# Both tiles' probabilities turned in one go, and small operations moved from VectorE to GpSimd, in an attention and MLP kernel

## The chip, the cores and the metric

One core of one Trainium2 chip runs the whole program. The metric is the device time of an execution in microseconds (us). Engines are PE (TensorE), VectorE (DVE in the rows), ScalarE (ACT), GpSimd (POOL) and SyncE (SP), which starts most transfers.

## The reference

```
scores = q @ k^T / 8                      # 4 batches x 8 heads, 576 x 576, head size 64
mask   = scores >= 32nd largest of the row
attn   = softmax(where(mask, scores, -1e9))
x      = (attn @ v) as 2304 tokens x 512
x      = softplus(x @ w_in) @ w_out       # 512 -> 2048 -> 512
logits = x @ w_gate                       # 8 experts, the largest one is taken
out    = gate * (relu(x @ w1[e]) @ w2[e]) # 512 -> 1024 -> 512 for the tokens of e
```

All of it is float32. Products whose result must be exact enough are made of three matmuls of a high and a low part of each operand (hi x hi, hi x lo, lo x hi); the low part is what is left when the rounded high part is subtracted.

## The kernel before, in words

Attention is cut into 72 blocks. A full block holds 128 queries of a pair of heads, so it has two tiles t = 0, 1 of 128 x 576 scores; a block of the kind "ends" collects the last 64 rows of two batches. Each engine has its program written out by hand, in steps i. In step i PE makes the scores of block i + 1, turns the probabilities of block i - 2 (transposes through PSUM, `turn_probs`) and multiplies them with v (`times_v`). VectorE finds the 32 largest values of block i by four rounds of MAX8 with a MATCH_REPLACE8 in between (`maxima`, `strike`) and makes the reciprocals of the softmax denominators (`reciprocals`). GpSimd masks block i - 1: one tile takes two operations (L1479, L1482), the other takes one on ScalarE (L848) and one on GpSimd (L1475). ScalarE copies scores out of PSUM (`scores_out`), takes exponentials (`exponentials`, L855), normalises (L861) and copies the turned tiles (`probs_out`, L868) and the product with v (`x_out`, L875), which is the high part of x; VectorE subtracts it from the PSUM value for the low part (`x_low`, L1128).

From step 10 (MLP_AT) to step 73 the first MLP runs beside attention: a group of 256 tokens takes eight units, one a step. `up` makes 256 features (24 matmuls, L598 to L600), ScalarE takes the absolute value, the rectified value and a logarithm (L883 to L892), GpSimd adds them (`softplus`, L1487), ScalarE copies the high part (`h_high`, L900), GpSimd subtracts for the low part (`h_low`, L1493), and in the next step `down` multiplies with w_out in two halves of six matmuls (L617 to L619). When a group is through, ScalarE empties the two banks of down (`down_out`), and in two steps of the next group (TURNS) PE turns a tile of tokens (`turn_tokens`) and computes its logits (`logits`), both in bank 5, which `up` uses too; `up` of the next step waits until the logits have been copied.

PSUM has 8 banks of 512 columns. Scores of a tile lie as two halves of 288 columns in two banks, four banks in all; the turned probabilities of one tile (640 columns) lie in the upper part of banks 0 to 4, the product with v in bank 4. There is room for one turned tile, so PE turns t = 0, makes half of down, waits for ScalarE's copy, and turns t = 1. After step 73 come the last MLP group, routing and the experts.

What orders the work is the sequence of calls in each engine's program; between engines stand semaphores.

Of the kernel before, what the change touches and what calls it, by code (L numbers as in the profile page):

```python
# [20 lines left out]
def build(nc, q, k, v, w_in, w_out, w_gate, w1, w2, out):  # L21
# [62 lines left out]
    TURNS = {}  # L84
# [32 lines left out]
    with ExitStack() as ctx:  # L117
# [35 lines left out]
        prT = phase("prT", [P, FULL + 1, 2, P])  # L153
# [3 lines left out]
        top = phase("top", [P, 6, TOPK])  # L157
        bias = phase("bias", [P, 2, 2, 2])
        den = phase("den", [P, 2, 2])
        rden = phase("rden", [P, 2, 2])  # L160
        phase("gap_b", [P, WLEN - 4 * PAIRS * SEQ // 2 - PAIRS * (FULL + 1) * P - 6 * TOPK - 3 * 8])
# [116 lines left out]
        first_scores = sem("first_scores")  # L278
# [5 lines left out]
        transit_full, transit_copied = sem("transit_full"), sem("transit_copied")  # L284
        pv_ready, x_copied, x_split = sem("pv_ready"), sem("x_copied"), sem("x_split")
# [48 lines left out]
        def x_source(n):  # L334
            raw = psum[:, 4, 0:P]
            return raw if PLAN[n][0] == "full" else raw.rearrange("p (t q) -> p t q", t=2)
# [173 lines left out]
        def _(pe):  # L510
            turns = 0

            def scores(n):
# [6 lines left out]
                if n >= 4:  # L520
                    pe.wait_ge(transit_copied, 2 * (n - 3))

                order = [(0, 0), (1, 0), (0, 1), (1, 1)] if n == 0 else [(0, 0), (0, 1), (1, 0), (1, 1)]
                for part, t in order:
                    keys = slice(part * HALF, (part + 1) * HALF)
                    for h in range(2):
# [7 lines left out]
                        mm = nc.tensor.matmul(psum[rows, 2 * part + t, 0:HALF],  # L534
                                              qT[h * HD:(h + 1) * HD, p, cols],
                                              kT[h * HD:(h + 1) * HD, p, keys],
                                              start=True, stop=True)
                    if n == 0 and (part, t) == (1, 0):
                        mm.then_inc(first_scores, 1)
                mm.then_inc(scores_ready, 1)  # L540

            def turn_probs(n, t):
                pe.wait_ge(pr_ready, 2 * n + t + 1)
                if n or t:
                    pe.wait_ge(transit_copied, 2 * n + t)
                if t == 0:
                    pe.wait_ge(scores_copied, 2 * min(n + 4, BLOCKS))
                if n and t == 0:
                    pe.wait_ge(x_copied, n)
                    pe.wait_ge(x_split, n)  # L550
                for c, keys in enumerate(KEYS):
                    mm = nc.tensor.transpose(transit[0:keys, c, :],  # L552
                                             pr[:, n % 2 * 2 + t, c * P:c * P + keys], ident[:])
                mm.then_inc(transit_full, 1)

            def times_v(n):
# [4 lines left out]
                pe.wait_ge(transit_copied, 2 * n + 2)  # L561
                for t, p in enumerate(pairs_of(n)):
                    for c, keys in enumerate(KEYS):
                        for h in range(2):
                            if kind == "full":
                                cols, probs = slice(0, P), prT[0:keys, c, h, :]
                            else:
                                cols = slice(t * HD, (t + 1) * HD)
                                probs = prT[0:keys, c, t, h * HD:(h + 1) * HD]
                            mm = nc.tensor.matmul(psum[h * HD:(h + 1) * HD, 4, cols],  # L570
# [3 lines left out]

            def up(g, u, amid=()):
                n = UNITS * g + u

                steps_x = PAIRS * 2 * (g + 1)
                k_last = KD - 1 if PIECES[2 * g + 1][0] == "full" else KD // 2
# [6 lines left out]
                if turns:  # L586
                    pe.wait_ge(logits_copied, turns)
                ps = psum[:, 5, 0:2 * WIDE].rearrange("p (a c) -> p a c", a=2)
                for part in range(2):
                    f = slice(part * P, (part + 1) * P)  # L590
                    for kk in range(KD):
                        if (part, kk) in amid:
                            amid[part, kk]()
                        if u == 0 and (part, kk) == (0, k_last):
                            pe.wait_ge(x_split, steps_x)
# [27 lines left out]
            def turn_tokens(g, kk, bank):  # L623
                pe.wait_ge(y_copied, kk + 1)
# [1009 lines left out]
```

## Time and profile before

| what | value |
| --- | --- |
| median of 3 runs | 1081.61 us (1079.75 to 3335.12) |
| the profiled execution | 1081.47 us |
| its span, first to last instruction | 1079.7 us |
| mean granted PE clock | 0.975 of full speed |
| PE, weight loads | 1006.0 us (93%), 810.3 us (75%) |
| VectorE | 842.9 us (78%) |
| ScalarE | 738.1 us (68%) |
| GpSimd | 651.6 us (60%) |

The busy times are unions over the whole span. The span has an opening without the MLP (to about 113 us), the stage with attention and MLP together (to about 768 us), and the last MLP group with routing and experts. So a share of the whole says little about one stage.

### The profile page before, as it was taken

To read this page: it belongs to the slowest core of one execution; us is meant where nothing else is said; L and a number is where in the kernel's file an instruction comes from. 1 tells how busy PE (TensorE), PEld (TensorE's weight loads), DVE (VectorE), ACT (ScalarE), POOL (GpSimd) and SP (SyncE) were. 2 spreads that over 40 slices of the span, in tenths; PEclk is the share of its full clock that TensorE was granted. 3 is DMA by queue.
4 is the path that set the end of the run, shared out by engine and by line. 5 is a ranking of instruction groups with operands and counts; after the bars stand their busy time and mean duration, and the time that the engine had idled before them with its cause. 6 is when DMAs were issued, how large, how long until landed. Compare 5 with 4: busy or idle time off the path is not lost.

```text
span 1079.7 us, 21621 instructions
## 1 busy us (share of the span) xinstructions
PE 1006.0 (93%) x6951; PEld 810.3 (75%) x6952; DVE 842.9 (78%) x1879; ACT 738.1 (68%) x1391; POOL 651.6 (60%) x624
## 2 busy tenths in 40 slices
PE   3566899999999999999999999999999999999996
PEld 1344678887787787787778887787887788888875
DVE  7999999999999999999999999997154622222261
ACT  2887788988988988988888988988646121111140
POOL 2678687777777877878868778778443302211101
PEclk9966899999999999999999999999999999999999
DMA  9623126343234443332444323233482331111100
GB/s 321 239 87 140 70 96 205 121 140 118 98 118 154 161 126 125 116 118 86 152 150 152 119 102 118 98 119 117 139 325 102 121 125 41 49 48 39 39 19 19
DMA packets 42110, 130.46 MB, mean 121 GB/s; under 512 B 4064, under 2 KB 17376, under 8 KB 31776
## 3 DMA queue, kind: packets, MB, share of 16 engines
q1 hardware_dynamic: 38976, 119.57, 31.4%
q0 software_dynamic: 3040, 9.70, 2.6%
q8 instruction: 52, 0.85, 0.3%
q14 instruction: 42, 0.34, 0.1%
HBM read 111.43 MB, written 18.09 MB: 120 GB/s over the span
## 4 chain that ended last, share of the span: by engine, by line
PE 52%; POOL 25%; ACT 10%; issue 9%; DMA 1%; SPq 1%; DVE 1%; ACTq 0%; POOLq 0%; DVEq 0%
POOL pr L1479 7%; PE psum L690 6%; PE psum L692 6%; PE psum L691 6%; PE psum L570 6%; POOL pr L1482 5%; POOL h_lo L1493 4%; PE psum L534 4%; POOL hs L1487 4%; POOL pr L1475 4%; PE psum L552 4%; PE psum L598 3%; PE psum L617 3%; PE psum L619 3%; PE psum L618 2%
## 5 line engine op out<-in xcount | busy, mean ns | idle before, releaser
L1116 DVE MAX8 top<-work 128x8 f32<-128x576 f32 x432 | 305.1, 748 | 0.0
L1122 DVE MATCH_REPLACE8 work<-top,work 128x576 f32<-128x576 f32 x288 | 212.0, 744 | 0.0
L598 PE MATMUL psum<-x_parts,wi_hi 128*128 128x256 f32 x576 | 170.8, 296 | 0.0
L1487 POOL TENSOR_TENSOR hs<-hs,ab 128x512 f32<-128x512 f32 x72 | 92.9, 1290 | 124.1 <-ACT ab L892 124.1
L599 PE MATMUL psum<-x_parts,wi_hi 128*128 128x256 f32 x576 | 163.5, 284 | 0.0
L600 PE MATMUL psum<-x_parts,wi_lo 128*128 128x256 f32 x576 | 163.5, 284 | 0.0
L1479 POOL TENSOR_SCALAR pr<-sc,top 128x576 f32<-128x576 f32 x64 | 142.6, 2228 | 6.4
L552 PE MATMUL psum<-ident,pr 128*128 128x128 f32 (+1 forms) x720 | 109.3, 285 | 37.2 <-ACT prT L868 16.2
L552 PEld LDWEIGHTS psum<-ident,pr 128*128 128x128 f32 (+1 forms) x720 | 77.4, 139 | 69.5 <-issue 69.5
L598 PEld LDWEIGHTS psum<-x_parts,wi_hi 128*128 128x128 f32 x576 | 110.7, 192 | 25.2 <-issue 23.8
L855 ACT ACTIVATE pr<-pr,bias 128x576 f32<-128x576 f32 x144 | 111.1, 772 | 26.9 <-POOL pr L1482 25.9
L570 PE MATMUL psum<-prT,vtok 128*64 128x128 f32 (+3 forms) x1600 | 117.1, 287 | 10.2 <-ACT prT L868 10.1
L617 PE MATMUL psum<-wo_ring,h_hi 128*128 x288 | 124.2, 431 | 1.0 <-POOL h_lo L1493 0.8
L1475 POOL TENSOR_TENSOR pr<-sc,pr 128x576 f32<-128x576 f32 x80 | 113.8, 1426 | 17.1 <-ACT pr L848 17.1
L570 PEld LDWEIGHTS psum<-prT,vtok 128*64 128x64 f32 (+1 forms) x1600 | 85.7, 144 | 50.6 <-issue 31.9
L534 PE MATMUL psum<-kT,qT 64*128 64x288 f32 (+1 forms) x640 | 110.4, 468 | 9.8 <-ACT sc L840 9.0
L619 PE MATMUL psum<-wo_ring,h_lo 128*128 x288 | 113.8, 395 | 0.0
L1577 POOL DMA_INDIRECT out<-ys,dst_now x19 | 19.2, 1012 | 156.6 <-DVE ys L1323 155.6
L618 PE MATMUL psum<-wo_ring,h_hi 128*128 x288 | 113.2, 393 | 0.0
L599 PEld LDWEIGHTS psum<-x_parts,wi_hi 128*128 128x128 f32 x576 | 111.0, 193 | 0.2
L600 PEld LDWEIGHTS psum<-x_parts,wi_lo 128*128 128x128 f32 x576 | 110.9, 193 | 0.0
L868 ACT COPY prT<-psum 128x640 f32<-128x640 f32 x144 | 99.7, 693 | 12.8 <-PE psum L552 12.8
(205 smaller groups left out, 2192.4 us busy)
## 6 DMA issues: line engine op xcount, KB each, us to landing
wo_ring<-wo_parts SPq DMA_DIRECT2D x72, 1024.0 KB, 4.9
wo_parts<-wo_ring SPq DMA_DIRECT2D x8, 1024.0 KB, 3.9
kT<-in_k SPq DMA_DIRECT2D x16, 288.0 KB, 3.6
qT<-in_q SPq DMA_DIRECT2D x16, 288.0 KB, 4.6
vtok<-in_v SPq DMA_DIRECT2D x16, 256.0 KB, 2.8
wo_raw<-in_moe_w_out SPq DMA_DIRECT2D x1, 4096.0 KB, 14.8
wi_raw<-in_moe_w_in SPq DMA_DIRECT2D x4, 1024.0 KB, 13.7
x_rows<-x2tok SPq DMA_DIRECT2D x16, 256.0 KB, 2.4
```

Of the source, the lines that this page charges most:

```text
L534: mm = nc.tensor.matmul(psum[rows, 2 * part + t, 0:HALF], qT[h * HD:(h + 1) * HD, p, cols], kT[h * HD:(h + 1) * HD, p, keys], start=True, ...
L552: mm = nc.tensor.transpose(transit[0:keys, c, :], pr[:, n % 2 * 2 + t, c * P:c * P + keys], ident[:])
L570: mm = nc.tensor.matmul(psum[h * HD:(h + 1) * HD, 4, cols], vtok[0:keys, p, c, h * HD:(h + 1) * HD], probs, start=(c == 0), stop=(c == FULL))
L598: nc.tensor.matmul(ps[:, part, :], wi_hi[:, u, kk, f], hi, start=first, stop=False)
L599: nc.tensor.matmul(ps[:, part, :], wi_hi[:, u, kk, f], lo, start=False, stop=False)
L600: mm = nc.tensor.matmul(ps[:, part, :], wi_lo[:, u, kk, f], hi, start=False, stop=last)
L617: nc.tensor.matmul(psum[:, 6 + a, :], high, hi, start=(f == 0), stop=False)
L619: mm = nc.tensor.matmul(psum[:, 6 + a, :], low, hi, start=False, stop=(f == KF - 1))
L1116: nc.vector.max(top[:, at, 8 * r:8 * r + 8], sc[:, at, :] if r == 0 else work[:, t, :]).then_inc(topk_step, 1)
L1122: nc.vector.match_replace(work[:, t, :], top[:, at, 8 * r - 8:8 * r], sc[:, at, :] if r == 1 else work[:, t, :], TAKEN).then_inc(topk_step, 1)
L1475: nc.gpsimd.tensor_tensor(to, sc[:, at, :], to, ALU.subtract).then_inc(masked, 1)
L1479: nc.gpsimd.tensor_scalar(to, sc[:, at, :], top[:, at, TOPK - 1:TOPK], OUT, ALU.is_lt, ALU.mult).then_inc(mask_step, 1)
```

## The change

- PSUM: a tile's scores are now 512 columns in a bank of its own (banks 0 and 1), and the last 64 keys of both tiles lie together in the first 128 columns of bank 2 (`ends`). The turned probabilities of both tiles (1280 columns) lie without a gap in banks 2 to 4, and the product with v in the last 128 columns of bank 4.
- PE turns both tiles one behind the other and then makes both halves of down. ScalarE copies both turned tiles in one instruction.
- The tokens are turned in bank 0 and the logits made in bank 1, in steps of their own: two tiles take four steps. In the first step of a group the scores stand in the middle of `up`.
- ScalarE copies the product with v to a buffer in SBUF (`xraw`), at the start of the next step; GpSimd makes the high part by a copy and the low part by a subtraction (`x_split_up`).
- The sum of the two parts of a denominator goes to GpSimd from block 9 on (`denominators`); the reciprocal stays on VectorE, one round of MAX8 later.
- ScalarE takes both exponentials behind the logarithm.
- The first block's scores are no longer copied in a separate first half.

```diff
-        transit = psum[:, 0:FULL + 1, HALF:HALF + P]
+        ends = psum[:, 2, 0:2 * REST]
+        transit = psum[:, 2:5, :].rearrange("p b c -> p (b c)")[:, P:P + 2 * (FULL + 1) * P]
+        x_raw_at = psum[:, 4, 3 * P:4 * P]
+        chunks = transit.rearrange("p (t c q) -> p t c q", t=2, c=FULL + 1)
...
-            TURNS[up_step(g) + UNITS + 1 + a] = (g, 2 * g + a)
+            TURNS[up_step(g) + UNITS + 1 + 2 * a] = (g, 2 * g + a)
+            LOGITS[up_step(g) + UNITS + 2 + 2 * a] = 2 * g + a
...
                 if late:
-                    turn_probs(i - 2, 0)
+                    turn_probs(i - 2)
+                if i in TURNS:
+                    turn_tokens(*TURNS[i], 0)
+                if i in LOGITS:
+                    logits(LOGITS[i], 1)
                 if down_at(i):
-                    down(*down_at(i), 0)
-                if late:
-                    turn_probs(i - 2, 1)
-                if i in TURNS:
-                    turn_tokens(*TURNS[i], 5)
-                if down_at(i):
-                    down(*down_at(i), 1)
+                    for part in range(2):
+                        down(*down_at(i), part)
                 if late:
                     times_v(i - 2)
-                if i in TURNS:
-                    logits(TURNS[i][1], 5)
...
+            def x_split_up(n):
+                pool.wait_ge(x_copied, n + 1)
+                g = PLAN[n][4] // 2
+                if g >= 2:
+                    pool.wait_ge(h_raw, UNITS * (g - 1))
+                nc.gpsimd.tensor_copy(x_place(0, n), x_source(n)).then_inc(x_hi_ready, 1)
+                pool.wait_ge(x_hi_ready, n + 1)
+                nc.gpsimd.tensor_tensor(x_place(1, n), x_source(n), x_place(0, n).bitcast(F32),
+                                        ALU.subtract).then_inc(x_split, 1)
+
+            def denominators(n):
+                pool.wait_ge(exp_ready, 2 * n + 2)
+                if n >= 2:
+                    pool.wait_ge(rden_ready, n - 1)
+                nc.gpsimd.tensor_tensor(den[:, n % 2, :], eps[:, n % 2, :, 0], eps[:, n % 2, :, 1],
+                                        ALU.add).then_inc(den_step, 1)
...
+                if i >= MLP_AT and is_block(i - 3):
+                    x_split_up(i - 3)
                 if up_at(i - 1):
                     h_low(*up_at(i - 1))
...
+                if is_block(i - 1) and i - 1 >= MLP_AT - 1:
+                    denominators(i - 1)
```

## Rows read from the trace of the kernel before

**Rows 1.** Busy time of each engine by stage, with granted clock and transfers.
```profile
core 0: us, PE busy (x) PEld busy (x) DVE busy (x) ACT busy (x) POOL busy (x), PEclk, DMA share, GB/s
118.00:750.00 632.00, 620.85 (x4934) 502.15 (x4933) 619.32 (x1408) 559.47 (x1086) 494.68 (x430) 1.00 0.36 124
311.91:393.64 81.73, 80.22 (x619) 64.81 (x618) 80.89 (x185) 72.93 (x143) 64.47 (x57) 1.00 0.41 139
```

**Rows 2.** Timeline of VectorE: start and duration in us, line, operation.
```profile
370.38 1.41 DVE L1116 MAX8 top<-work 128x8 f32<-128x576 f32 x2
...
380.03 0.15 DVE L1133 TENSOR_REDUCE den<-eps 128x2 f32<-128x4 f32 x1
380.21 0.17 DVE L1136 RECIPROCAL rden<-den 128x2 f32<-128x2 f32 x1
380.29 0.27 DVE L1128 TENSOR_TENSOR x_parts<-psum,x_parts 128x128 fp32r<-128x128 f32 x1
380.48 1.41 DVE L1116 MAX8 top<-work 128x8 f32<-128x576 f32 x2
```

**Rows 3.** Timeline of PE's matmuls, one step with tokens and logits.
```profile
298.60 1.24 PE L534 MATMUL psum<-kT,qT 64*128 64x288 f32 x8
...
302.75 0.71 PE L552 MATMUL psum<-ident,pr 128*128 128x128 f32 x5
303.22 0.48 PE L617 MATMUL psum<-wo_ring,h_hi 128*128 x1
303.54 0.39 PE L618 MATMUL psum<-wo_ring,h_hi 128*128 x1
...
304.46 0.40 PE L619 MATMUL psum<-wo_ring,h_lo 128*128 x1
304.77 0.74 PE L552 MATMUL psum<-ident,pr 128*128 128x128 f32 x5
305.35 0.60 PE L628 MATMUL psum<-ident,x2tok 128*128 128x128 f32 x4
305.71 0.48 PE L617 MATMUL psum<-wo_ring,h_hi 128*128 x1
...
307.27 1.46 PE L570 MATMUL psum<-prT,vtok 128*64 128x128 f32 x20
308.66 1.06 PE L638 MATMUL psum<-wg,x2T 128*128 128x8 f32 x8
309.65 1.24 PE L534 MATMUL psum<-kT,qT 64*128 64x288 f32 x8
```

**Rows 4.** Timeline of GpSimd, one step; in brackets the idle time before and its releaser.
```profile
403.69 2.23 POOL L1479 TENSOR_SCALAR pr<-sc,top 128x576 f32<-128x576 f32 x1
406.00 1.43 POOL L1482 TENSOR_TENSOR pr<-pr,sc 128x576 f32<-128x576 f32 x1
407.38 1.44 POOL L1475 TENSOR_TENSOR pr<-sc,pr 128x576 f32<-128x576 f32 x1
410.24 1.28 POOL L1487 TENSOR_TENSOR hs<-hs,ab 128x512 f32<-128x512 f32 x1 [1.42 <-ACT ab L892]
411.60 0.23 POOL L1465 TENSOR_SCALAR bias<-top 128x2 f32<-128x2 f32 x1
...
412.25 1.30 POOL L1493 TENSOR_TENSOR h_lo<-hs,h_hi 128x512 fp32r<-128x512 f32 x1
413.65 2.23 POOL L1479 TENSOR_SCALAR pr<-sc,top 128x576 f32<-128x576 f32 x1
```

**Rows 5.** Timeline of ScalarE in the same step.
```profile
407.52 0.78 ACT L855 ACTIVATE pr<-pr,bias 128x576 f32<-128x576 f32 x1 [0.51 <-POOL pr L1482]
...
408.30 0.67 ACT L868 COPY prT<-psum 128x640 f32<-128x640 f32 x1
...
411.55 0.62 ACT L900 CAST h_hi<-hs 128x512 fp32r<-128x512 f32 x1 [0.48 <-POOL hs L1487]
```

**Rows 6.** Waits of GpSimd from 118 to 750 us: total, times, longest.
```profile
POOL hs L1487 <- ACT ab L892: 100.9, 62, 2.9
```

**Rows 7.** Groups by line and shape: count, busy us, mean ns, idle before.
```profile
L1509 POOL TENSOR_SCALAR_AFFINE_SELECT ident<-ident 128x128 f32<-128x128 f32 x1 | 0.3, 288 | 0.2 <-POOL ident L1507 0.2
L1504 POOL TENSOR_TENSOR wi_lo<-wi_raw,wi_hi 128x1024 fp32r<-128x1024 f32 x8 | 18.9, 2364 | 0.0
```

More of the change, by code:

```diff
@@ L510, in _ @@
         def _(pe):
-            turns = 0
+            turns, logit_turns = 0, 0
             def scores(n):
@@ L520, in scores @@
                 if n >= 4:
[L521 to L525, printed above, removed]
+                    pe.wait_ge(transit_copied, n - 3)
+                if turns:
+                    pe.wait_ge(turn_copied, turns)
+                if logit_turns:
+                    pe.wait_ge(logits_copied, logit_turns)
+                for last, t in ((True, 0), (False, 1), (False, 0), (True, 1)):
+                    keys = slice(FULL * P, SEQ) if last else slice(0, FULL * P)
+                    to = ends[:, t * REST:(t + 1) * REST] if last else psum[:, t, :]
+                    if last and t:
+                        pe.wait_ge(ends_begun, n + 1)
                     for h in range(2):
@@ L533, in scores, with turn_probs @@
                             rows = slice(h * HD, (h + 1) * HD)
[L534 to L535 removed]
+                        mm = nc.tensor.matmul(to[rows, :], qT[h * HD:(h + 1) * HD, p, cols],
                                               kT[h * HD:(h + 1) * HD, p, keys],
                                               start=True, stop=True)
[L538 to L539 removed]
+                    if last and t == 0:
+                        mm.then_inc(ends_begun, 1)
                 mm.then_inc(scores_ready, 1)
[L542 to L548, printed above, removed]
[L549 to L554 removed]
+            def turn_probs(n):
+                if n:
+                    pe.wait_ge(transit_copied, n)
+                    pe.wait_ge(x_copied, n)
+                pe.wait_ge(scores_copied, 2 * min(n + 4, BLOCKS))
+                for t in range(2):
+                    pe.wait_ge(pr_ready, 2 * n + t + 1)
+                    for c, keys in enumerate(KEYS):
+                        mm = nc.tensor.transpose(chunks[0:keys, t, c, :],
+                                                 pr[:, n % 2 * 2 + t, c * P:c * P + keys], ident[:])
+                    mm.then_inc(transit_full, 1)
             def times_v(n):
@@ L573, in times_v, with k_last @@
                 mm.then_inc(pv_ready, 1)
+            def k_last(g):
+                return KD - 1 if PIECES[2 * g + 1][0] == "full" else KD // 2
             def up(g, u, amid=()):
@@ L593, in up @@
                             amid[part, kk]()
-                        if u == 0 and (part, kk) == (0, k_last):
+                        if u == 0 and (part, kk) == (0, k_last(g)):
                             pe.wait_ge(x_split, steps_x)
@@ L1007, in _ @@
                         exponentials(i - 1, 0)
-                    if late:
-                        probs_out(i - 2, 1)
-                    if now:
                         exponentials(i - 1, 1)
@@ L1018, in _ @@
                     h_high(*up_at(i - 1))
+                if is_block(i - 3):
+                    x_out(i - 3)
+                if now:
+                    for t in cuts(i - 1):
+                        cut_off(i - 1, t)
                 if is_block(i + AHEAD):
-                    scores_out(i + AHEAD, 0)
-                    scores_out(i + AHEAD, 1)
+                    scores_out(i + AHEAD)
                 if late:
@@ L1024, in _ @@
                     normalise(i - 2, 1)
-                if now:
-                    for t in cuts(i - 1):
-                        cut_off(i - 1, t)
                 if up_at(i):
@@ L1030, in _ @@
                 if late:
-                    probs_out(i - 2, 0)
-                if now and i < BLOCKS:
-                    exponentials(i - 1, 0)
-                if late:
-                    probs_out(i - 2, 1)
-                if now and i >= BLOCKS:
-                    exponentials(i - 1, 0)
+                    probs_out(i - 2)
                 if i in TURNS:
-                    turn_out(TURNS[i][1], 5)
+                    turn_out(TURNS[i][1], 0)
+                if i in LOGITS:
+                    logits_out(LOGITS[i], 1)
                 if up_at(i):
```

117 lines of the change are left out of this document (56 added, 61 removed).

## The prediction

> **What bounds the kernel now.** I read the table by stage first, because the shares of the whole span mix three stages. In the stage in which attention and the first MLP run together (118 to 750 us) VectorE is busy 619.32 of 632 us, PE 620.85, ScalarE 559.47, GpSimd 494.68, with the clock at 1.00 (2.4 GHz) throughout [rows 1]. So two engines are full and no single one is "the" bound. The stage is 64 steps in eight rounds of eight; the second row is one round, 81.73 us, a mean step of 10.22 us. The last stage is experts, which the change leaves alone: all the change can earn lies in these 64 steps and the ten before them.
>
> Next I read each engine's own sum over one step, its pure work without waits.
>
> VectorE: from one MAX8 pair at the same place in the code to the next, 370.38 to 380.48, is 10.10 us with nothing idle [rows 2]. Eight of them are 80.8 us of the round's 81.7.
>
> PE: the step from 298.60 to 309.65 is packed, 11.05 us [rows 3]. In it scores and up take 4.15, the first turn 0.47, six matmuls of down 1.55, the second turn 0.58 (with the seam before the tokens, which I take at 0.08), the tokens' transposes 0.36, the second down 1.56, the product with v 1.39 and the logits 0.99. Without tokens, logits and that seam a step is 9.62. Two steps in eight carry them: 8 x 9.62 + 2 x 1.43 = 79.8 us.
>
> GpSimd and ScalarE: together they close a loop. From the mask's start at 403.69 the two mask operations release the exponential at 407.52 (ScalarE); a copy at 408.30 and the two halves of the logarithm follow it there; these release the sum at 410.24, it releases the copy at 411.55, that one the subtraction at 412.25, and the next mask starts at 413.65: 9.96 us [rows 4, 5]. GpSimd itself waits in this loop, 100.9 us over 62 steps for the logarithm [rows 6]. Eight turns are 79.7 us.
>
> So the ceilings of a round are 80.8 (VectorE), 79.8 (PE) and 79.7 (the loop), and the round takes 81.73: 0.9 above the highest. The three are within 1.4%; this is the fact on which the forecast rests. Relieving one of them earns no more than the distance to the next.
>
> **The change part by part.** *VectorE loses* the sum of the denominators and the low part of x; the reciprocal stays. Its rows start at 380.03, 380.21, 380.29 and 380.48 [rows 2]: the sum is worth 0.18 us, the low part 0.19. The step falls from 10.10 to 9.73, the round to 77.8. The reciprocal now sits behind a wait for GpSimd; queued behind it are four MAX8 and two strikes of the block, some 4.1 us, and GpSimd needs their result only for the biases, nearly a step later. I cost this at nothing; without the cover each 0.1 us of lateness is 0.1 us a step.
>
> *GpSimd gains* a copy of x (128x128), a subtraction (128x128) and a two-column add. The subtraction: 2364 ns at 1024 columns [rows 7] against 1.43 us at 576 (406.00) [rows 4] gives 2.1 ns a column over a fixed 0.22, so 0.49 at 128. The copy does not occur in this form. From below it is bounded by that fixed part, 0.2, from above by the rate of the TENSOR_SCALAR at 403.69 (2.23 us for 576 columns, about 3.5 ns each over a fixed 0.2), 0.66; the nearest row is the one-input select over 128x128, 0.29 [rows 7], and I take 0.30. The small add is taken at a bias operation, 0.23 (411.60). Each gets a seam of 0.07, as between the end of one operation (403.69 + 2.23) and the start of the next (406.00). GpSimd's own sum for a step is then copy 0.37, subtraction 0.56, low part of h 1.40 (412.25 to 413.65), mask 2.31 + 1.38 + 1.44, softplus 1.36 (410.24 to 411.60), biases 0.60 (0.65 up to 412.25, less a short wait), add 0.30: 9.72 us. Before the change it was 8.5 and hidden; now it stands at the same height as VectorE. In the step in which ScalarE also empties the down banks (two copies, 1.05 us) the copy of x comes some 0.4 later. Round: 8 x 9.72 + 0.4 = 78.2, with bounds from 76.9 (copy 0.10 and add 0.06 cheaper) to 82.9 (copy at 0.66, add at twice its price).
>
> One rule speaks against this choice of engine. The Trainium skill, GPSIMD Engine Reference, section "When to use GPSIMD", advises VectorE for elementwise work, saying that GpSimd is about half as fast on two inputs and near line rate on one. By that the copy would be an estimated 0.31 us and the step about 9.73. Its advice holds for an engine with time to spare; the trace has VectorE without any, and no row here shows the copy.
>
> *The loop through the logarithm is cut.* Both exponentials now come after it on ScalarE, so softplus on GpSimd runs beside them. What closes the loop is new: the second exponential, the copy of h's high part, the copy of x out of PSUM, then the two x operations, low h and three mask operations on GpSimd, and the exponential again: an estimated 0.75 + 0.58 + 0.31 (ScalarE, near the 0.78 and 0.62 of [rows 5]) + 0.93 + 1.40 + 5.13 + 0.09 = 9.2 us, less than GpSimd's own 9.72. So the latter counts.
>
> *PE* turns both tiles in one go and does both down halves in one go. Inside a half of down the matmuls follow each other at 0.23 us (303.54 to 304.46 in four), so six are 1.38 and the 1.55 hold 0.17 of seams between the two kinds of matmul [rows 3]. One such pair goes, and the wait for the copy between the tiles with it: I take 0.15 a step, bounds 0.05 and 0.25. The scores keep their columns (4 x 288 become 2 x 512 + 2 x 64) and their alternation of the two halves of the rows; bounds of -0.05 and +0.2 for eight weight loads over short columns, taken at 0. The logits move to steps of their own and no longer wait in the same step for their copy. Round: 79.8 - 1.2 = 78.6, bounds 77.4 and 81.0. But steps with logits are now 10.5 us, with tokens 9.9, against 9.5 in the others: four long steps in a row make PE late by about 1.7 us against GpSimd. The others can take about 0.9 of it. This is an estimate: if E is the end of the second exponential, ScalarE has both tiles normalised at E + 4.4 and PE asks for the second 4.6 after the start of its step, so PE can't start before E - 0.2; on the late side ScalarE wants up's result at E + 4.4, 4.2 after that start, and has 0.5 to spare, so E + 0.7. The rest, 0.8, is lost once a round.
>
> *ScalarE*: one copy of 1280 columns in place of two of 640 (0.67 at 408.30 [rows 5]) saves 0.15; an additional short copy of scores costs the same. It is busy 559.47 of 632 [rows 1], 8.9 us a step, and stays under the others; its new waits in order (softplus, both turned tiles, two masks) have 0.8 us of room.
>
> *The first ten steps* have no MLP, and I take VectorE as their bound too; the low part of x leaves 7 of them: -1.3 us (0 if something else binds there). The first tile's scores are no longer brought out ahead: +0.3 us. The x of a new group must now pass through two GpSimd operations before the first up; the scores put in the middle of that up (1.2 us) cover it, and what is left over, up to 0.4 a round, is in the 0.8 above.
>
> **The sum.** Highest ceiling 78.6, loss through the uneven steps 0.8, and 0.5 for the three ceilings lying within 0.8 of each other: 79.9 us a round in place of 81.73. Eight rounds: -14.6. With -1.3 and +0.3: -15.6. The profiled execution took 1081.47 us (span 1079.7), the median of the runs shown is 1081.61, so 1066 us. By the bounds above a round lies between 78.3 (GpSimd at its forecast, nothing lost) and 83.4 (GpSimd at its upper bound plus 0.5): 1053 to 1094 us.
>
> **Rivals.** (a) *GpSimd becomes the bound and the kernel gets slower.* Its step is one chain in order, and the copy of x waits for ScalarE's copy out of PSUM. With the copy at 0.66, the add at 0.44 and 0.4 us of idle for x_raw in each step it is 10.7 us; a round 85.6 + 0.9, so 8 x 4.8 - 1.0, +37 us: 1119 us. It decides from a step of 10.22 us on, and 2% are lost at 10.57. For it: GpSimd had 8.5 us and gets 1.2 more, in the loop. Against: the select row. Chance 0.06. (b) *PE is the bound.* The short score matmuls cost 0.2 us more, which eats the seams saved: round 80.2 + 0.9 = 81.1, -6 us in all: 1076 us. Chance 0.22. (c) *The ties dissolve*: seams of 0.25, no loss by uneven steps: a round of 78.3, 28 us less in all, 1053 us. Chance 0.25. (d) *The change doesn't relieve VectorE*, which waits for GpSimd's sum as long as it summed itself: the step stays 10.1, 1080 us. For it: VectorE already waited for the exponentials in some steps; against: 4 us of room. Chance 0.05. The forecast, 1061 to 1072 us, has 0.42.
>
> **How the numbers follow.** 2% (21.6 us) is about what a measurement here can tell from no change. Faster by over 2% asks for under 1060 us, a round of 79.1 or less: (c) and the lower edge of the forecast, 0.28. Slower by over 2% is the upper part of (a), 0.05. The rest, 0.67, is within. The range takes in (b), (c), (d) and the near end of (a): and leaves out the top of the bounds: 1050 to 1090 us.
>
> **What would show it.** VectorE should be the engine with idle time, about 0.3 us or more a step before the reciprocal; its step without waits 9.73. GpSimd should be busy over 9.2 of 10 us, its wait for the logarithm nearly gone. PE should show 12 down matmuls in a row and a step of about 9.5 between waits. A GpSimd copy above 0.45 us, or ScalarE idle for more than 0.8 us a step in front of its copies, would prove the forecast wrong upwards; rounds under 79 us downwards.

## The result

| kernel | median, us | runs |
| --- | --- | --- |
| before | 1079.86 | 1079.57 to 1081.61, beside one of 3335.12 |
| changed | 1074.18 | 1073.49 to 1075.62, 5 runs |

The ratio is 0.9943, with a 95% interval of 0.9931 to 0.9955: 6 us less. The forecast was 16 us less. The run of 3335.12 us stands apart and is left out of the comparison. The profiled executions are 1081.47 and 1073.49 us, with spans of 1079.7 and 1071.3; that of before is at the upper end of its runs and that of the changed kernel at the lower, so the 8.4 us between the spans are more than the medians show.

The busy times of the changed kernel (us, share of the span, instructions) and its mean granted clock by slice:

```profile
span 1071.3 us, 21596 instructions
...
PE 1002.0 (94%) x6952; PEld 831.1 (78%) x6953; DVE 818.3 (76%) x1744; ACT 737.9 (69%) x1390; POOL 712.7 (67%) x831
...
PEclk9755899999999999999999999999999999999999
```

By stage, in the columns of [rows 1]: the first ten steps, the stage with attention and MLP, and a stretch as long as one round.

```profile
10.00:110.00 100.00, 56.21 (x288) 40.60 (x284) 91.47 (x203) 69.76 (x124) 65.91 (x62) 0.69 0.49 176
118.00:750.00 632.00, 627.34 (x5012) 526.65 (x5009) 602.62 (x1297) 569.88 (x1101) 559.04 (x624) 1.00 0.36 125
287.15:367.01 79.86, 79.73 (x618) 67.27 (x617) 78.02 (x170) 73.19 (x143) 71.45 (x81) 1.00 0.40 143
```

The first row of before for the same 100 us, which did not stand above:

```profile
10.00:110.00 100.00, 56.67 (x306) 36.04 (x304) 97.54 (x218) 73.80 (x128) 66.10 (x52) 0.80 0.54 194
```

Against [rows 1] PE is busy 6.5 us more of the same 632, VectorE 16.7 less, GpSimd 64 more. But in the opening VectorE has dropped from 97.54 to 91.47 us of 100. Its waits for ScalarE's exponentials in that stretch:

```profile
DVE den L1131 <- ACT pr L868: 8.3, 8, 1.3
```

Before they were two waits in the same 100 us, 2.0 us in all, and 0.4 us of that from 40 us on.

To see where the time went I took the start of the product with v (L570 before, L581 after) of each block from the timelines. The distance between two of them is the length of a step.

| stretch | before | after | difference |
| --- | --- | --- | --- |
| up to the product of the first block | 37.4 | 35.7 | -1.7 |
| from there to that of block 9 | 94.5 | 100.3 | +5.8 |
| block 9 to block 71 | 634.2 | 622.0 | -12.2 |
| from there to the end | 313.6 | 313.3 | -0.3 |

Some 1 us of the first row is a transfer of weights that landed earlier in that execution. The next table has typical steps of the opening and, in their order, those of one round. Measured from product to product, tokens fall on the first and second step of the round before and logits on the second and third; after the change tokens fall on the second and fourth, logits on the third and fifth.

| steps, us | before | after |
| --- | --- | --- |
| opening | 10.17, 10.17, 10.09 | 11.25, 11.24, 11.25 |
| one round | 10.79, 11.06, 10.60, 9.60, 9.82, 9.94, 9.96, 9.97 | 10.11, 10.06, 10.50, 10.02, 10.50, 9.57, 9.55, 9.56 |
| its sum | 81.7 | 79.9 |

So the round came out as forecast to 0.1 us, and the opening went the other way. What follows asks why the opening got longer, what bounds the round now, and what had bounded it before.

In the profile the forecast prices can be checked too. GpSimd's two operations on x, by line and shape:

```profile
L1473 POOL TENSOR_TENSOR x_parts<-xraw,x_parts 128x128 fp32r<-128x128 f32 x72 | 32.9, 458 | 5.8
L1471 POOL CAST x_parts<-xraw 128x128 fp32r<-128x128 f32 x72 | 20.9, 290 | 25.8 <-ACT xraw L887 21.3
```

The copy takes 290 ns where I took 0.30 us. The Trainium skill, GPSIMD Engine Reference, section "When to use GPSIMD", has one-input operations near line rate, an estimated 0.31 us; the trace agrees.

One step of PE after the change, with tokens, to be read beside [rows 3]:

```profile
309.98 1.35 PE L548 MATMUL psum<-kT,qT 64*128 64x64 f32 x8
...
311.25 0.39 PE L609 MATMUL psum<-x_parts,wi_hi 128*128 128x256 f32 x1
...
314.23 1.25 PE L563 MATMUL psum<-ident,pr 128*128 128x128 f32 x10
315.32 0.60 PE L641 MATMUL psum<-ident,x2tok 128*128 128x128 f32 x4
315.68 0.48 PE L628 MATMUL psum<-wo_ring,h_hi 128*128 x1
...
318.62 1.46 PE L581 MATMUL psum<-prT,vtok 128*64 128x128 f32 x20
320.00 1.35 PE L548 MATMUL psum<-kT,qT 64*128 64x64 f32 x7
```

Read from start to start: scores 1.27 (1.17 before), up 2.98, both turns 1.09, tokens 0.36, twelve matmuls of down 2.94 (3.11 before), the product 1.38. There is no gap in it: this is PE's own sum.

### The profile page after: what moved, and what is told of

The parts are those of the page before. It is cut to its first block, busy times and chain, and to the rows that moved or that the text cites. A ratio compares the mean times of both kernels' runs of the same rounds, so it can differ in the third digit from the quotient of the medians.

```text
span 1071.3 us, 21596 instructions
## 1 busy us (share of the span) xinstructions
PE 1002.0 (94%) x6952; PEld 831.1 (78%) x6953; DVE 818.3 (76%) x1744; ACT 737.9 (69%) x1390; POOL 712.7 (67%) x831
## 4 chain that ended last, share of the span: by engine, by line
PE 84%; ACT 6%; DVE 3%; issue 3%; DMA 1%; POOL 1%; SPq 1%; ACTq 0%; DVEq 0%; POOLq 0%
PE psum L581 8%; PE psum L563 8%; PE psum L609 8%; PE psum L548 7%; PE psum L702 6%; PE psum L704 6%; PE psum L703 6%; PE psum L610 6%; PE psum L611 6%; PE psum L628 6%; PE psum L630 6%; PE psum L629 6%; PE psum L734 2%; DMA wo_raw<-in_moe_w_out 1%; PE psum L651 1%
## 5 line engine op out<-in xcount | busy, mean ns | idle before, releaser
L581 PE MATMUL psum<-prT,vtok 128*64 128x128 f32 (+3 forms) x1600 | 117.1, 287 | 12.2 <-ACT prT L881 12.2
L563 PE MATMUL psum<-ident,pr 128*128 128x128 f32 (+1 forms) x720 | 99.6, 290 | 30.4 <-ACT sc L853 26.9
L581 PEld LDWEIGHTS psum<-prT,vtok 128*64 128x64 f32 (+1 forms) x1600 | 85.6, 144 | 52.0 <-issue 41.7
L548 PE MATMUL psum<-kT,qT 64*128 64x64 f32 (+3 forms) x640 | 116.0, 480 | 9.4 <-ACT sc L853 8.8
L628 PE MATMUL psum<-wo_ring,h_hi 128*128 x288 | 118.8, 413 | 1.0 <-POOL h_lo L1506 0.9
L629 PE MATMUL psum<-wo_ring,h_hi 128*128 x288 | 112.7, 391 | 0.0
L548 PEld LDWEIGHTS psum<-kT,qT 64*128 64x128 f32 (+1 forms) x640 | 74.0, 193 | 49.4 <-issue 44.5
L563 PEld LDWEIGHTS psum<-ident,pr 128*128 128x128 f32 (+1 forms) x720 | 82.6, 143 | 35.9 <-issue 24.8
```

The costliest lines, as they stand in the source:

```text
L548: mm = nc.tensor.matmul(to[rows, :], qT[h * HD:(h + 1) * HD, p, cols], kT[h * HD:(h + 1) * HD, p, keys], start=True, stop=True)
L563: mm = nc.tensor.transpose(chunks[0:keys, t, c, :], pr[:, n % 2 * 2 + t, c * P:c * P + keys], ident[:])
L581: mm = nc.tensor.matmul(x_raw_at[h * HD:(h + 1) * HD, cols], vtok[0:keys, p, c, h * HD:(h + 1) * HD], probs, start=(c == 0), stop=(c == FULL))
L628: nc.tensor.matmul(psum[:, 6 + a, :], high, hi, start=(f == 0), stop=False)
L629: nc.tensor.matmul(psum[:, 6 + a, :], high, lo, start=False, stop=False)
```

## The experiments

Times are medians; the ratio is to the kernel before on the same chip, with its 95% interval. "Round" is the sum of eight steps from the timeline.

| run | median, us | ratio to before | round, us |
| --- | --- | --- | --- |
| changed kernel | 1074.18 | 0.9943 (0.9931 to 0.9955) | 79.9 |
| a1, other order in the opening | 1067.63 | 0.9877 (0.986 to 0.9893) | 79.9 |
| a2, scores ahead of up | 1071.51 | 0.9914 (0.9897 to 0.993) | 79.3 |
| a3, sum on VectorE | 1074.09 | 0.9938 (0.9921 to 0.9954) | 79.9 |
| a4, light PE | 1046.73 | 0.9688 (0.9671 to 0.9705) | 77.4 |
| a5, VectorE at its old load | 1085.70 | 1.0052 (1.0034 to 1.0071) | 81.8 |
| a6, logits together | 1075.87 | 0.9963 (0.9949 to 0.9978) | 80.0 |
| a7, exponential before the logarithm | 1093.04 | 1.0124 (1.0102 to 1.0146) | 82.8 |
| a8, tiles turned apart | 1094.55 | 1.0139 (1.0117 to 1.0161) | 82.8 |
| b1, before without the sum | 1080.94 | 1.0 (0.999 to 1.001) | 81.7 |
| b2, before with light PE | 1076.26 | 0.9956 (0.9939 to 0.9973) | 81.7 |
| b3, before, logarithm first | 1076.17 | 0.9956 (0.9939 to 0.9972) | 80.9 |
| c1, a1 and a2 | 1063.71 | 0.9846 (0.9832 to 0.9859) | 79.3 |

### Why the opening got longer: a1_early_order

ScalarE in one opening step of the changed kernel, from the normalising to the copy of the turned tiles:

```profile
72.59 1.44 ACT L874 ACTIVATE pr<-pr,rden 128x576 f32<-128x576 f32 x2
...
74.08 1.44 ACT L861 ACTIVATE pr<-sc,bias 128x576 f32<-128x576 f32 x2
75.42 0.26 ACT L850 ACTIVATE sc<-psum 128x128 f32<-128x128 f32 x1
75.58 1.07 ACT L853 ACTIVATE sc<-psum 128x512 f32<-128x512 f32 x2
79.31 1.23 ACT L881 COPY prT<-psum 128x1280 f32<-128x1280 f32 x1 [2.66 <-PE psum L563]
80.43 1.05 ACT L918 CAST wo_ring<-wo_raw 128x1024 fp32r<-128x1024 f32 x1
```

The same part in the kernel before:

```profile
75.52 0.69 ACT L868 COPY prT<-psum 128x640 f32<-128x640 f32 x1 [0.98 <-PE psum L552]
76.11 1.05 ACT L906 CAST wo_ring<-wo_raw 128x1024 fp32r<-128x1024 f32 x1
...
77.05 0.78 ACT L855 ACTIVATE pr<-pr,bias 128x576 f32<-128x576 f32 x1
...
77.82 0.68 ACT L868 COPY prT<-psum 128x640 f32<-128x640 f32 x1
```

In the opening of the changed kernel PE's transposes take longer than later: ten span 2.37 us where they span 1.25 to 1.34 in the MLP stage. In the step shown of the kernel before, ScalarE waited 0.98 us for five of them and did other work while PE turned the second tile. Now it stands idle 2.66 us for all ten, with the weight copy and two exponentials queued behind it. The edit only moves that work ahead of the wait:

```diff
-                    if late:
-                        probs_out(i - 2)
                     if wo_unit(i) is not None:
                         split_wo(wo_unit(i))
                     if now:
                         exponentials(i - 1, 0)
+                    if late:
+                        probs_out(i - 2)
+                    if now:
                         exponentials(i - 1, 1)
```

> The changed kernel, but in the first ten steps ScalarE makes the weight copy and the first exponential before it copies the turned probabilities, so that PE's ten transposes run beside them. Theory (turning both tiles in one go leaves ScalarE idle for all ten slow transposes, 2.7 us a step, where it waited 1 us for five): the early step falls from 11.25 us to about 10.3 us, some 7 us in all, 1067 us. Rival (the early steps are long because the granted clock is lower there, 0.69 in 10 to 110 us against 0.80 before): the step stays at 11.25 us and the time at 1074 us.

1067.63 us, 6.5 below the changed kernel. ScalarE:

```profile
82.20 1.06 ACT L918 CAST wo_ring<-wo_raw 128x1024 fp32r<-128x1024 f32 x1
83.14 0.80 ACT L868 ACTIVATE pr<-pr,bias 128x576 f32<-128x576 f32 x1
...
84.99 1.23 ACT L881 COPY prT<-psum 128x1280 f32<-128x1280 f32 x1 [0.96 <-PE psum L563]
```

The wait is 0.96 us and the step 10.27; from the first product to that of block 9 it takes 92.5 us, 7.8 less than the changed kernel and 1.9 less than before. The rival is answered by the granted clock of the same 20 us (80 to 100) in the two kernels, first the changed one, then a1:

```profile
80.00:100.00 20.00, 13.01 (x69) 9.44 (x70) 17.43 (x39) 16.48 (x30) 14.74 (x14) 0.50 0.26 106
```

```profile
80.00:100.00 20.00, 14.24 (x77) 10.38 (x75) 19.66 (x45) 16.89 (x30) 17.94 (x17) 0.50 0.24 100
```

Both have 0.50 (1.2 GHz) there, and the steps are 11.25 and 10.27. So the order alone is worth 1 us a step at the same granted clock. That the lower mean clock of the opening (0.69 against 0.80) adds nothing to the difference from the kernel before is not shown by this, because before, the transposes were quick in some steps and slow in others:

```profile
74.74 0.74 PE L552 MATMUL psum<-ident,pr 128*128 128x128 f32 x5 [1.45 <-issue]
...
84.82 1.30 PE L552 MATMUL psum<-ident,pr 128*128 128x128 f32 x5 [1.45 <-issue]
...
87.00 1.30 PE L552 MATMUL psum<-ident,pr 128*128 128x128 f32 x5 [0.87 <-ACT prT L868]
```

The step with both tiles slow (products at 78.56 and 89.20) took 10.64 us, the usual one 10.17. In the changed kernel the ten are slow in each step from 31.89 to 99.40. With quick ones ScalarE's wait of 2.66 us would be some 1.1 shorter (an estimate from 2.37 and 1.25), so the longer step needs the merged turn and the slow transposes together; no run here has the changed order with quick ones. The order is the part that an edit can take away.

### The scores inside up: a2_no_amid

```diff
-                if up_at(i) and up_at(i)[1] == 0 and is_block(i + AHEAD):
-                    amid[0, k_last(up_at(i)[0])] = lambda: scores(i + AHEAD)
-                elif is_block(i + AHEAD):
+                if is_block(i + AHEAD):
                     scores(i + AHEAD)
```

> The changed kernel, but with the scores ahead of up in the first step of a group too, as in every other step. Theory (that step, 10.11 us against 9.56, is long through the seams of a split up, 0.27, and because ScalarE gets the scores 1.3 us late and PE then waits 0.3 for the normalised tile; the x of the group is ready 0.8 us before PE would ask): the step falls to 9.6 us, a round to 79.3, some 4 us in all, 1070 us. Rival (the placement covers the detour of x over GpSimd, as the prediction had it): PE now waits for x and the step stays at 10.1 us or grows; 1074 us or more.

1071.51 us, 2.6 below the changed kernel. The step falls from 10.11 to 9.56 in every round, so the detour of x over GpSimd needed no cover: a part of the change that cost 0.55 us a round for a wait that isn't there. In the profiled executions the stretch from block 9 to block 71 takes 618.2 us against 622.0, which is the 7 x 0.55 of the theory. The medians show 2.6 of it; the runs of each kernel spread over some 2 us.

### What bounds the round after the change: a3, a4, a5

a3 gives the sum back to VectorE:

```diff
-                if n < MLP_AT - 1:
-                    dve.wait_ge(exp_ready, 2 * n + 2)
-                    nc.vector.tensor_reduce(...).then_inc(den_step, 1)
+                dve.wait_ge(exp_ready, 2 * n + 2)
+                nc.vector.tensor_reduce(...).then_inc(den_step, 1)
...
-                if is_block(i - 1) and i - 1 >= MLP_AT - 1:
-                    denominators(i - 1)
```

> The changed kernel with the sum of the denominators given back to VectorE in all steps. Theory (PE sets the round of 79.9 us now; VectorE's step would be 9.9 us, eight of them 79.3): no change of the round, at most 2 us in all. Rival (the relief of VectorE is what brought the round down): 0.18 us a step come back, 11 us, 1085 us.

1074.09 us. From block 12 on the steps are the same to 0.03 us; only the three behind block 9 are longer, 9.89 for 9.7. Moving the sum to GpSimd was worth nothing that the times show.

a4 leaves out the matmul of w_in's low part in up:

```diff
-                        nc.tensor.matmul(ps[:, part, :], wi_hi[:, u, kk, f], lo, start=False, stop=False)
-                        mm = nc.tensor.matmul(ps[:, part, :], wi_lo[:, u, kk, f], hi,
-                                              start=False, stop=last)
+                        mm = nc.tensor.matmul(ps[:, part, :], wi_hi[:, u, kk, f], lo,
+                                              start=False, stop=last)
```

> The changed kernel without the third matmul of up (low part of w_in times high part of x), which leaves out a correction of the first product; PE has about 0.95 us less a step. Theory (PE is the highest ceiling, GpSimd and VectorE stand 1.5 to 2 us a round under it): the round falls from 79.9 to about 78.3 us and no further, though PE loses 7.6 us of work in it; 12 us in 64 steps, and one more for each up outside them: 1061 us. Rival (the engines are tied to each other by the order of waits, not by one engine's sum): it falls by less than 0.5 us a round.

1046.73 us. The round falls to 77.4, and the stretch of one round reads:

```profile
319.80:397.20 77.40, 73.58 (x552) 59.18 (x551) 77.40 (x169) 72.36 (x143) 71.17 (x80) 1.00 0.49 162
```

VectorE is busy all of the 77.40 us (the rounds of this run take 76.6 to 77.7). Of the 7.6 us that PE lost a round, 2.5 came out: PE is the ceiling at 79.9. That VectorE is the next is read from its missing idle time; no run here makes VectorE lighter on top of this. The forecast's 77.8 for VectorE was right, mine for a4 (78.3) a little high. The total fell by 27 us where I expected 13: 4.5 in the last group, and more in the stretches with "ends" blocks, where PE has most to do (83.6 to 78.6 over the eight steps from block 48).

a5 puts VectorE back to its old load: the sum as in a3, and one subtraction of the same size as the low part of x, into a tile that nobody reads.

```diff
                         reciprocals(n - 2)
+                        nc.vector.tensor_tensor(spare[:], ident[:], ident[:], ALU.subtract)
```

> The changed kernel with VectorE at its old load: the sum of the denominators given back to it, and one subtraction over 128x128 a step whose result nobody reads, in place of the low part of x (which stays on GpSimd). VectorE's step is then about 10.1 us, eight of them 80.8. Theory (VectorE stands just under PE now; at its old load it would be above PE's 79.9 us a round): the round grows to about 80.8 us, 7 us in all, 1081 us. Rival (VectorE does not bind at any of these loads, as its relief brought nothing in the kernel before): 1074 us.

```profile
366.47 0.14 DVE L1131 TENSOR_REDUCE den<-eps 128x2 f32<-128x4 f32 x1
366.65 0.17 DVE L1134 RECIPROCAL rden<-den 128x2 f32<-128x2 f32 x1
366.73 0.27 DVE L1147 TENSOR_TENSOR spare<-ident 128x128 f32<-128x128 f32 x1
366.92 1.42 DVE L1118 MAX8 top<-work 128x8 f32<-128x576 f32 x2
```

1085.70 us, 11.5 above the changed kernel, and slower than the kernel before. The steps of a round are 9.56, 10.25, 10.12, 10.11, 10.49, 10.58, 10.03 and 10.67: against the changed kernel two of the three ordinary ones grow from 9.56 to VectorE's 10.1 or a little more, one with tokens from 10.04 to 10.49, and those with logits by 0.1 and 0.2 (the fourth, 10.11, is the one with the scores inside up and stays). The round is 81.8, not 80.8: one engine's long steps hardly make up for another's, nearly each step costs the larger of the two. So the relief of VectorE is needed, but half of it does: 9.9 a step (a3) is as good as 9.7, 10.1 is not.

### Which parts of the change carry the gain: a6, a7, a8

a6 puts tokens and logits of a tile back into one step, the logits behind the product with v in bank 5, where `up` waits for their copy:

```diff
-            TURNS[up_step(g) + UNITS + 1 + 2 * a] = (g, 2 * g + a)
-            LOGITS[up_step(g) + UNITS + 2 + 2 * a] = 2 * g + a
+            TURNS[up_step(g) + UNITS + 1 + a] = (g, 2 * g + a)
+            LOGITS[up_step(g) + UNITS + 1 + a] = 2 * g + a
...
-                if i in LOGITS:
-                    logits(LOGITS[i], 1)
...
                 if late:
                     times_v(i - 2)
+                if i in LOGITS:
+                    logits(LOGITS[i], 5)
```

> The changed kernel with tokens and logits of a tile in the same step again, the logits in bank 5 behind the product with v and ScalarE's copy of them at the end of the step, two steps a group. Theory (PE's own sum sets the round, and it doesn't change by the place of the logits): the round stays within 0.5 us of 79.9, 1074 to 1078 us. Rival (the gain of the change is that the chain from the logits over the scores and ScalarE back to the logits, 11.05 us in the kernel before, is broken up): the round goes back towards 81.7, 1085 us or more.

1075.87 us; the steps are 11.02 and 10.55 for the two, and the round 80.0 instead of 79.9. PE's sum doesn't care where they stand. "Logits over four steps" is worth 1.7 us by the medians and 1.3 us between blocks 9 and 71; the interval (0.9949 to 0.9978) overlaps that of the changed kernel, so even this is not clear of noise.

a7 puts one exponential ahead of the logarithm again:

```diff
+                if now:
+                    exponentials(i - 1, 0)
                 if up_at(i):
                     logarithm(*up_at(i))
                 if now:
-                    exponentials(i - 1, 0)
                     exponentials(i - 1, 1)
```

> The changed kernel with ScalarE's first exponential ahead of the logarithm again. Theory (this closes the loop mask, exponential, logarithm, softplus, high part, mask again, and GpSimd's new work on x lies in it: 3.8 + 0.8 + 1.3 + 1.4 + 0.6 + 0.3 + 0.8 + 1.4, about 10.4 us a step): the round grows to 83 us, 25 us in all, 1100 us. Rival (PE's sum hides it): 1074 us.

1093.04 us, 18.9 above the changed kernel; ordinary steps are 10.34 us, the 10.4 that the sum of the loop gave. The waits from 300 to 700 us name both of its halves, GpSimd for the logarithm and ScalarE for the mask (total, times, longest):

```profile
POOL hs L1501 <- ACT ab L904: 33.6, 39, 1.6
ACT pr L868 <- POOL pr L1496: 23.2, 36, 1.0
```

a8 turns the second tile between the two halves of down again, with one copy of both:

```diff
                 if late:
-                    turn_probs(i - 2)
+                    turn_probs(i - 2, (0,) if down_at(i) else (0, 1))
+                if down_at(i):
+                    down(*down_at(i), 0)
+                    if late:
+                        turn_probs(i - 2, (1,))
...
                 if down_at(i):
-                    for part in range(2):
-                        down(*down_at(i), part)
+                    down(*down_at(i), 1)
```

> The changed kernel, but PE turns the second tile between the two halves of down again; one copy of both tiles stays. Theory (PE is the ceiling and pays 0.16 us for one more pair of seams between kinds of matmul): 0.16 us a step, the round 81.2, 10 us in all, 1084 us. Rival (the seams are hidden behind the waits): 1074 us.

1094.55 us, 20.4 above the changed kernel where I expected 10. The seams are there, but the larger part is a wait that I had not seen:

```profile
ACT prT L885 <- PE psum L564: 50.2, 39, 1.4
```

ScalarE waits 1.3 us in each of 39 steps for the second tile behind half of down, with the logarithm and both exponentials queued behind the copy. One copy of both tiles asks for both turns in one go.

### What bounded the round before: b1, b2, b3

b1 takes the reciprocal of the sum that ScalarE leaves, without the reduction:

```diff
-                nc.vector.tensor_reduce(den[:, n % 2, :], eps[:, n % 2], AX.X, ALU.add
-                                        ).then_inc(den_step, 1)
-                dve.wait_ge(den_step, n + 1)
-                nc.vector.reciprocal(rden[:, n % 2, :], den[:, n % 2, :]).then_inc(rden_ready, 1)
+                nc.vector.reciprocal(rden[:, n % 2, :], eps[:, n % 2, :, 0]).then_inc(rden_ready, 1)
```

> The kernel before, with the reciprocal taken of the sum that ScalarE left, without VectorE's reduction; this leaves out only the addition of 1e-9. VectorE has 0.18 us less a step and no other engine has more. Theory (VectorE was the highest ceiling, 80.8 us of a round of 81.7, PE and the loop through the logarithm 1.0 lower): the round falls by about 1 us, 8 us in all, 1072 us. Rival (the loop of GpSimd and ScalarE alone set the pace and VectorE only followed): no change, 1080 us.

Nothing, with an interval of 0.1% to either side, and the same round of 81.7 us. The theory falls: VectorE, without any idle time over a whole step [rows 2], was not what set the pace.

b2 is the edit of a4 in the kernel before.

> The kernel before, without the third matmul of up (low part of w_in times high part of x), which leaves out a correction of the first product. PE has about 0.95 us less a step. Theory (VectorE at 80.8 us a round is the ceiling): the round falls by the 0.9 us that it stands above it, 7 us in all with the up of the last group, 1072 us. Rival (PE set the pace in the steps with tokens and logits, 11.05 us each): those fall by 0.95 each and more, the round by 2 us or more, 1062 us.

1076.26 us, but the round is 81.7, with the same 10.77, 11.05, 10.61, 9.6. What it gained lies behind the stage (4.0 us from the last product with v to the end). So PE's sum wasn't it either. ScalarE and PE in the step with tokens and logits:

```profile
298.44 1.24 PE L534 MATMUL psum<-kT,qT 64*128 64x288 f32 x8
...
299.73 1.19 ACT L839 ACTIVATE sc<-psum 128x576 f32<-128x576 f32 x2 [0.50 <-PE psum L534]
300.81 1.44 ACT L860 ACTIVATE pr<-pr,rden 128x576 f32<-128x576 f32 x2
...
303.76 0.70 ACT L867 COPY prT<-psum 128x640 f32<-128x640 f32 x1
...
304.61 0.73 PE L552 MATMUL psum<-ident,pr 128*128 128x128 f32 x5 [0.83 <-ACT prT L867]
305.18 0.60 PE L627 MATMUL psum<-ident,x2tok 128*128 128x128 f32 x4
...
307.11 1.46 PE L570 MATMUL psum<-prT,vtok 128*64 128x128 f32 x20
308.50 1.06 PE L637 MATMUL psum<-wg,x2T 128*128 128x8 f32 x8
309.49 1.24 PE L534 MATMUL psum<-kT,qT 64*128 64x288 f32 x8
```

PE has time now and waits for the copy of the first tile. From the scores at 298.44 over ScalarE's scores, normalising, cut, both halves of the rectifying and the copy of the first tile (until 304.5) to the second turn, tokens, half of down, the product, the logits and the next scores at 309.49 is a closed loop of 11.05 us. In the step behind, which has neither tokens nor logits, the same loop takes 9.62 (scores at 309.49 and 319.11). `up` is not in it, so making `up` shorter changes nothing. In [rows 3] this loop looked like PE's own sum, as its length happened to be the same.

b3 adds to b1 the order of the change on ScalarE, both exponentials behind the logarithm:

```diff
-                if now and i < BLOCKS:
-                    exponentials(i - 1, 0)
                 if late:
                     probs_out(i - 2, 1)
-                if now and i >= BLOCKS:
-                    exponentials(i - 1, 0)
...
                 if up_at(i):
                     logarithm(*up_at(i))
                 if now:
+                    exponentials(i - 1, 0)
                     exponentials(i - 1, 1)
```

> The kernel before, without VectorE's reduction (as in the run without the sum, which leaves out the addition of 1e-9), and with both exponentials behind the logarithm on ScalarE, as the change has them; the tiles are still turned one at a time. Theory (in ordinary steps the loop mask, exponential, logarithm, softplus, mask of 9.96 us sets the pace, in steps with logits the chain logits, scores, copies, second turn, down, product, logits of 11.05 us): the ordinary steps fall towards 9.7 us, the steps with logits stay at 11.05; some 6 us in all, 1074 us. Rival (ScalarE only waits elsewhere, for the second turn behind the first half of down): no gain or a loss, 1080 us or more.

1076.17 us. The ordinary steps go from 9.96 to 9.62, the ones with tokens and logits stay at 11.05 and even reach the one ahead of them (11.03). Both loops are where the theory has them. It is 4.2 us less than the kernel before beside it, where I expected some 6. The 9.62 has two readings that this run doesn't tell apart: it is PE's own sum for an ordinary step, and also the length of the second loop in a step without tokens and logits.

### The two edits that helped: c1_both

> The changed kernel with both edits that helped: the first exponential ahead of the copy of the turned tiles in the first ten steps, and the scores ahead of up in every step. Theory (one acts before 118 us, the other after it, so they add): 6.5 and 2.7 us less than the changed kernel, 1065 us. Rival (the earlier start of the stage is eaten by the rounds): 1068 us, as with the first edit alone.

1063.71 us, a ratio of 0.9846 (0.9832 to 0.9859): 17 us below the kernel before, the fastest of the versions that leave nothing out. The two edits add.

## Why the prediction was wrong, step by step

**The round** was forecast at 79.9 us and measured at 79.9. **The opening** is the step that failed: "The first ten steps have no MLP, and I take VectorE as their bound too; the low part of x leaves 7 of them: -1.3 us (0 if something else binds there)." Measured was +5.8 us from the first product to that of block 9. I had costed what leaves VectorE there and not the new order on ScalarE, and had given no row for the opening. With the order of a1 the kernel takes 1067.6 us, close to the 1066 forecast, and the stretch is 1.9 us shorter than before: the relief of VectorE had been priced about rightly, for an order that the kernel didn't have. The prediction had itself named the sign, ScalarE idle for more than 0.8 us a step in front of its copies; it was 2.66 us, in the opening. Between the profiled executions the 15.6 us of the forecast became 8.4: 7.1 us went in the opening, 2.4 in the 62 steps behind it, and 2.3 came back before the first product and at the end.

**The highest ceiling before** was read wrongly. The 80.8 us of VectorE did not bind (b1), nor did PE's 79.8 (b2). What did were two closed loops, 9.96 us over the logarithm, which I had, and 11.05 us over the logits, which I had taken for PE's sum. b3 takes the first away and leaves the second. After the change PE's sum is the ceiling (a4), as rival (b) had it, but with a round of 79.9 and not its 81.1; that its 1076 us lies near the measured time is an accident of the opening.

**VectorE's relief**: the durations were about right (in a4 it is busy without a gap through a round of 77.4, forecast 77.8). The sum's move earned nothing (a3); a full return costs 11.5 us (a5). The wait behind the reciprocal cost nothing, as forecast: VectorE waited for GpSimd's sum 22.5 us in 26 of the steps, time it had over.

```profile
DVE rden L1134 <- POOL den L1480: 22.5, 26, 5.8
```

**GpSimd's gain**: copy 290 ns for 0.30, subtraction 458 ns for 0.49, addition 193 ns for 0.23. Right. Its whole step was put a little too high: from mask to mask (342.90 to 352.47) it takes 9.57 us, not 9.72, and it is busy 71.45 of 79.86 us, 8.9 of 10 where I had named over 9.2. So rival (a) is out. Its waits for the logarithm fell from 100.9 us [rows 6] to 21.0.

```profile
POOL hs L1500 <- ACT ab L904: 21.0, 35, 1.5
```

**PE**: I had -0.15 a step for the seams and 0 for the scores. Down takes 2.94 for 3.11, but the scores 1.27 for 1.17 (within my bounds of -0.05 and +0.2). The ordinary step is 9.56 where I had 9.47. The loss of 0.8 a round through uneven steps did not occur; 0.55 was lost to the scores inside up (a2), which I had taken for a cover. So the round came out right by luck, by a sum whose terms were each off by some tenths and offset each other: 79.3 of PE's own and 0.55, for 78.6, 0.8 and 0.5. The 0.9 us by which I let the other engines give way to PE's uneven steps is small by a5.

**The number of rounds**: I took eight alike. From block 9 on the 62 steps gave 12.2 us, not 14.6. In the stretches with the "ends" blocks the steps of the changed kernel are 0.4 to 0.8 us longer, and the gain is 1 us or less: 84.6 to 83.6 over the eight steps from block 48.

**The range** (1050 to 1090) and the sign held; the size did not, 6 us for 16.

A general point on reading: the Trainium skill, Trainium Kernel Development and Optimization, section "Best Practices", says of the distance to the roofline that matmul busy time is a poor measure and that for other engines occupancy will do. That is not yet what sets the pace. PE was busy 80.22 of 81.73 us [rows 1] and a lighter PE changed no step of the round (b2), in line with the first half. VectorE was busy 80.89 of 81.73, so hardly idle, and its relief changed nothing either (b1): its occupancy did not name the bound.

## What to carry to other kernels

When several engines seem full, don't compare their sums only: write down each closed chain of waits through the order of the instructions, with its length, for each kind of step; two of three ceilings did not bind here. Whoever merges two turns and their copies into one makes the reader wait for both: look at what is queued behind that wait in every stage, above all in one where the producer is slower. And check each stage with a row of its own, even a short one: ten steps took back nearly half of what sixty-two had earned.

## What was not expected of the hardware

The same ten transposes take 2.4 us in the opening and 1.25 to 1.34 in the MLP stage, and the granted clock alone doesn't tell them apart: in the changed kernel they take 2.40 at 31.89 us, in a stretch with a granted clock of 1.00 (2.4 GHz), and 2.36 at 54.41, in one of 0.50 (1.2 GHz). The two timeline rows, then the two stretches:

```profile
31.89 2.40 PE L563 MATMUL psum<-ident,pr 128*128 128x128 f32 x10 [8.68 <-ACT sc L853]
...
54.41 2.36 PE L563 MATMUL psum<-ident,pr 128*128 128x128 f32 x10 [2.45 <-ACT sc L853]
```

```profile
30.00:40.00 10.00, 6.71 (x38) 5.10 (x38) 9.46 (x21) 7.51 (x14) 5.57 (x5) 1.00 0.96 326
...
46.00:60.00 14.00, 9.21 (x54) 6.98 (x54) 12.01 (x25) 11.35 (x20) 10.60 (x10) 0.50 0.19 77
```

Why they are as slow where the records grant the full clock stays open; no run here was made for it. In the MLP stage PE has hardly a gap in front of them, in the opening it has been idle for over 2 us. But idle time alone doesn't decide it either: after 1.45 us of it five transposes of the kernel before took 0.74 us at 74.74 and 1.30 at 84.82, and in a1, after 1.56 us each time, ten took 1.28 us at 63.03 and 2.37 at 72.32. Nor do whole executions follow the mean granted clock: three of a1 with 0.997 took 1067.5 to 1068.1 us, the one with 0.975 took 1066.3.
